# Products of constants in the waits of attention's tail and of the routing, and the sum of the MLP's lists moved into the first chunk

## The chip, the cores and the metric

The kernel runs on one core of one Trainium2 chip. A core has TensorE (matrix products into PSUM), VectorE, ScalarE and GpSimd, and queues that issue transfers (SyncE's above all). The engines run on their own and meet at semaphores. The metric is the device time of one launch in microseconds. Before the change it is 556.07 us, the median of three runs (555.29 to 556.83).

## The reference

Three layers, one behind the other, in float32:

```
attention: 2 batches, 8 heads, 768 positions, 64 wide; a position sees the first n_sink (4) keys
           and the last window (128); softmax; result as x[1536, 512]
experts:   tokens with x @ w_skip > 0 go to the expert e = argmax(x @ w_gate) of 8:
           x + p[e] * relu(x @ w1[e]) @ w2[e]        w1: 512 x 1024, w2: 1024 x 512
           the other tokens pass unchanged
MLP:       h = x @ w_in (512 x 2048); g = h if h > 0 else exp(h) - 1; out = g @ w_out
```

## The kernel before

**Attention** works on pairs of heads: 8 pairs times 6 tiles of 128 queries are 48 units (`UNITS`). TensorE's program for a unit u transposes its probabilities (`turn_unit`), makes the scores of unit u+2 (`qk`), at times transposes packed sinks (`turn_sinks`) and a finished block of x (`turn_x`), multiplies a block with the gate weights (`gate`), and does the products with the values of unit u-1 (`pv`). ScalarE and VectorE copy the transposed tiles from PSUM. Four more steps (`STEPS` = 52) drain this pipeline: in steps 46 and 47 no scores are left to make, in steps 50 and 51 only the last two gate products and the last transpose are left. Unit 0 and 1 already have fills (`early_fill`, L1403): products of a bf16 tile of ones with itself, 512 columns wide, into a PSUM tile that nobody reads.

**Routing** is a relay. VectorE finds each token's expert (`hot_b`); TensorE counts tokens per expert and ranks them (L1554 to L1562); VectorE turns ranks into slots, and for each of 12 token tiles makes a one-hot tile `here`; TensorE sums with it which token stands in each row of chunk 0 (L1571 to L1576), GpSimd gathers that chunk's rows into `xg`. VectorE then classifies tokens, TensorE ranks the classes (L1577 to L1585, for the order in which the MLP will read its rows), VectorE makes 12 more tiles `here`, and TensorE sums the other chunks' lists (L1587 to L1592). A chunk is 128 rows of one expert.

**Experts.** `turn(g)` transposes the gathered rows of chunk g, ScalarE copies them to `xg_t`. `chunk` (L1603) does 64 instructions of the up block (8 tiles of 128 hidden values, in float32), transposes the next chunk's rows, and does 24 products of the down block (each weight and each activation split into a high and a low part, three products each). In the first chunk the gates are summed between the up block and the transposes (`sum_gates`). Behind the first chunk, TensorE loads from memory how many chunks the first expert has, runs a loop over them if there is a second, and then sums the lists for the MLP: for 9 tiles, 18 products of `there` (a one-hot tile made by VectorE) into `ps_list`, which VectorE copies after chunk 0 (`keep_lists`, L1300). Then comes expert 1 (`expert(0, 1)`), which loads its first and last chunk and loops.

**The MLP** follows, in 4 blocks of 3 tiles.

The order on every engine is the order of its program text; nothing is scheduled at run time but the loops over chunks.

Of the kernel before, what the change touches and what calls it, by code (L numbers as in the profile page):

```python
# [22 lines left out]
def build(nc, q_t, k_s, v_p, n_sink, window, w_skip, w_gate, w1, w2, w_in, w_out, out):  # L23
# [86 lines left out]
    with ExitStack() as ctx:  # L110
# [1263 lines left out]
        def _(pe):  # L1374
# [41 lines left out]
            with pe.If(fits > 0):  # L1416

                def turn_unit(u):

                    pe.wait_ge(prob_ready, 2 * u + 2)  # L1420
                    if u >= 1:

                        pe.wait_ge(turned_a, u)
                        pe.wait_ge(turned_b, u)
                    if x_turned_at(u - 1) is not None:
                        pe.wait_ge(xt_kept, x_turned_at(u - 1) + 1)
                    if gate_at(u - 1) is not None:
                        pe.wait_ge(gate_added, gate_at(u - 1) + 1)
                    for h in range(2):
                        for m, (_, c) in enumerate(key_tiles(u % QT)):  # L1430
                            last = pe.transpose(ps_turn[h][:, m, :], prob_of(u, h)[:, c:c + P], identity[:])  # L1431
                    last.then_inc(unit_turned, 1)
# [50 lines left out]
                def sinks_pv(g):  # L1483

                    if g == 1:
# [3 lines left out]
                    pe.matmul(ps_pv[g % 2][:, 0:2 * PV], sink_t[:], v_sink[:, g // PG].rearrange("p i d -> p (i d)"),  # L1489
                              start=False, stop=True, skip_group_check=True).then_inc(group_done, 1)  # L1490

                for u in range(STEPS):
                    if u < 2:
                        early_fill(3 + u)
                    if u < UNITS:
                        turn_unit(u)
                    if u + 2 < UNITS:
                        qk(u + 2)
                    g = sinks_turned_at(u)
                    if g is not None:  # L1500
                        turn_sinks(u, g)
                    if gate_at(u) is not None:
                        gate(u, gate_at(u))
                    if x_turned_at(u) is not None:
                        turn_x(u, x_turned_at(u))
                    if 1 <= u <= UNITS:
                        pv(u - 1)
                    if g is not None:
                        sinks_pv(g)
            with pe.Else():  # L1510
# [27 lines left out]
                with pe.Fori(0, NT) as t:  # L1538
# [8 lines left out]
                                         start=(c == 0), stop=(c == DC - 1))  # L1547
                    last.then_inc(logits_ready, 1)

            pe.wait_ge(route_step, HOT)  # L1550
            pe.wait_ge(const_done, 9)
            rank = ps_rank[:, 0:NT * E].rearrange("p (t e) -> p t e", e=E)
            for t in range(NT):
                last = pe.matmul(ps_count[0:E, 0:NT], hot_b[:, t, :], ones[:, 0:NT], start=(t == 0), stop=(t == NT - 1))  # L1554
# [1 line left out]
            for t in range(NT - 1):  # L1556
                pe.matmul(rank[:, t + 1:, :], ones[:], hot_b[:, t:t + 1, :].broadcast_to([P, NT - 1 - t, E]),
                          start=(t == 0), stop=False, skip_group_check=True)
            pe.matmul(rank, tri[:], hot_b[:], start=False, stop=False, skip_group_check=True)
            pe.wait_ge(rows_ready, 1)  # L1560
            pe.matmul(ps_rank[:, 0:NT * E + E1], rows_b[0:E, :], below_b[0:E, :], start=False, stop=True,
                      skip_group_check=True).then_inc(ranks_ready, 1)  # L1562
# [2 lines left out]
            def turn(g):  # L1565
# [2 lines left out]
                    last = pe.transpose(ps_x[:, c, :], xg[:, c * P:(c + 1) * P], identity[:])  # L1568
                last.then_inc(xg_turned, 1)

            for t in range(NT):  # L1571
                pe.wait_ge(here_ready, t + 1)
                for m in range(2):
                    last = pe.matmul(ps_source[:, 0:1], here[:, t, :], token_id[:, m, t, :],
                                     start=(t == 0 and m == 0), stop=(t == NT - 1 and m == 1))
            last.then_inc(sources_summed, 1)  # L1576
            pe.wait_ge(order_step, CLASSED)  # L1577
            for t in range(ET - 1):
                pe.matmul(ps_place[:, t + 1:, :], ones[:], member[:, t:t + 1, :].broadcast_to([P, ET - 1 - t, E1]),
# [2 lines left out]
            for t in range(ET):  # L1582
                last = pe.matmul(ps_place, ones[:], lower[:, t:t + 1, :].broadcast_to([P, ET, E1]),
                                 start=False, stop=(t == ET - 1), skip_group_check=True)
            last.then_inc(places_ranked, 1)  # L1585
            pe.wait_ge(first_named, 1)
            for t in range(NT):  # L1587
                pe.wait_ge(here_ready, NT + t + 1)
                for m in range(2):
                    last = pe.matmul(ps_source[:, 0:CHUNKS], here[:, t, :], named[:, m, t, :],  # L1590
                                     start=(t == 0 and m == 0), stop=(t == NT - 1 and m == 1))
            last.then_inc(sources_summed, 1)  # L1592
            pe.wait_ge(routed, 1)
            pe.sem_inc(down_done, 1)
            turn(0)
            def sum_gates():
                pe.wait_ge(gates_named, 1)
                for t in range(NT):
                    last = pe.matmul(ps_gates[:, 0:3 * CHUNKS], here[:, t, :], gates_as[:, :, t, :],
                                     start=(t == 0), stop=(t == NT - 1))  # L1600
                last.then_inc(gates_summed, 1)

            def chunk(pair, half, g, first=False):  # L1603
                at = DOWN_AT[half]
# [7 lines left out]
                    last.then_inc(up_done, 1)  # L1612
                if first:
                    sum_gates()

                turn(g + 1)
                pe.wait_ge(y_copied, g + 1)
# [17 lines left out]
            with pe.If(second > 1):  # L1635
                with pe.Fori(1, second) as g:
                    chunk(0, 0, g)
            for t in range(ET):
                pe.wait_ge(there_ready, t + 1)
                for m in range(2):  # L1640
                    last = pe.matmul(ps_list, there[:, t, :], listed_as[:, m, t].rearrange("p k j -> p (k j)"),
                                     start=(t == 0 and m == 0), stop=(t == ET - 1 and m == 1))
            last.then_inc(lists_summed, 1)
            expert(0, 1)
            with pe.Fori(1, E // 2) as pair:
                for half in range(2):
# [134 lines left out]
```

## Time and profile before

| | |
|---|---|
| median of 3 runs | 556.07 us (555.29 to 556.83) |
| the profiled execution's own time | 555.49 us |
| its span (first to last instruction) | 553.7 us |
| mean granted clock of TensorE | 0.985 |
| TensorE busy, products / weight loads | 533.0 us (96%) / 462.4 us (84%) |
| VectorE / ScalarE / GpSimd busy | 271.1 / 216.3 / 50.7 us |
| chain that ended last | TensorE 89%, DMA 3%, VectorE 3%, issue 2%, ScalarE 2% |

Attention ends at about 138 us, the routing at about 154 us, the experts at about 277 us; the rest is the MLP. In the profile PE is TensorE's products, PEld its weight loads, DVE VectorE, ACT ScalarE, POOL GpSimd, SP SyncE. Times are in us from the start of the span; a wait in brackets behind an instruction is its engine's idle time before it, with what ended it. "issue" is time in which nothing that the profile shows was waited for. Ends of products are modelled, so that the length of one in a row of many is longer than its share of the row.

### The profile page before, as it was taken

The page shows a single profiled execution, that of the slowest core. Times are in us where ns is not written, and L with a number is a line of the kernel's source. Part 1 is how long each engine was busy: PE and PEld are TensorE (multiplying, and loading weights), DVE is VectorE, ACT ScalarE, POOL GpSimd, SP SyncE. Part 2 cuts the span into 40 slices and gives each one's busy share as a digit, 9 for nine tenths or more (in the row PEclk, how much of TensorE's full clock was granted, in tenths as well). Part 3 has the DMA queues.
Part 4 walks back from the last instruction along what each step waited for, and adds up shares of the span by engine and source line. Part 5 has one row for each costly group of instructions (what it writes and reads, how often), then busy time and mean ns, then how long its engine had stood idle before and what let it go on. Part 6 is the DMA issues. An engine that isn't in the chain of part 4 may idle for free.

```text
span 553.7 us, 8991 instructions
## 1 busy us (share of the span) xinstructions
PE 533.0 (96%) x3270; PEld 462.4 (84%) x3271; DVE 271.1 (49%) x726; ACT 216.3 (39%) x429; POOL 50.7 (9%) x108
## 2 busy tenths in 40 slices
PE   8999999998599999999999999999999999999997
PEld 4777777777388998998989899999999999999996
DVE  6566655553884345555766634333343333433332
ACT  4566565553043334445644423322233222332222
POOL 6000000000111101111220000400004000020000
PEclk9999999999589999999999999999999999999999
DMA  9468997322118559999952000200003000010001
GB/s 211 139 237 286 306 302 245 117 93 97 40 40 323 204 192 343 360 358 343 369 186 76 1 0 1 99 16 1 1 1 114 0 0 0 1 57 1 1 0 57
DMA packets 46956, 72.22 MB, mean 130 GB/s; under 512 B 16452, under 2 KB 16708, under 8 KB 46916
## 3 DMA queue, kind: packets, MB, share of 16 engines
q1 hardware_dynamic: 42018, 61.35, 32.6%
q0 software_dynamic: 2400, 7.87, 4.5%
q10 hardware_dynamic: 2498, 2.51, 1.3%
q8 instruction: 21, 0.34, 0.2%
q14 instruction: 19, 0.16, 0.1%
HBM read 57.56 MB, written 14.16 MB: 130 GB/s over the span
## 4 chain that ended last, share of the span: by engine, by line
PE 89%; DMA 3%; DVE 3%; issue 2%; ACT 2%; ACTq 0%; POOL 0%; POOLq 0%; DVEq 0%
PE ps_out L1690 24%; PE ps_g L1379 24%; PE ps_h L1610 9%; PE ps_y L1379 7%; PE ps_pv L1477 7%; PE ps_qk L1400 5%; PE ps_turn L1431 4%; DMA xg<-rows,source_i 3%; PE ps_turn L1459 2%; PE ps_pv L1489 1%; DVE prob L1045 1%; PE ps_turn L1447 1%; PE ps_x L1568 1%; PE ps_turn L1439 1%; PE ps_x L1653 1%
## 5 line engine op out<-in xcount | busy, mean ns | idle before, releaser
L1379 PE MATMUL ps_g<-x_hi,w_hi 128*128 128x384 f32 x252 | 85.1, 338 | 0.0
L1379 PE MATMUL ps_g<-x_lo,w_hi 128*128 128x384 f32 x252 | 84.8, 336 | 0.0
L1379 PE MATMUL ps_g<-x_hi,w_lo 128*128 128x384 f32 x252 | 84.7, 336 | 0.0
L956 ACT ACTIVATE g_raw<-ps_g 128x384 f32<-128x384 f32 x64 | 31.5, 492 | 125.7 <-PE ps_g L1379 123.0
L1353 DVE TENSOR_SCALAR g_raw<-g_raw 128x384 f32<-128x384 f32 x64 | 23.1, 361 | 117.3 <-ACT g_raw L956 117.3
L1690 PE MATMUL ps_out<-w_hi,g_hi 128*128 128x512 f32 x192 | 75.5, 393 | 0.2
L1690 PE MATMUL ps_out<-w_hi,g_lo 128*128 128x512 f32 x192 | 75.5, 393 | 0.0
L1690 PE MATMUL ps_out<-w_lo,g_hi 128*128 128x512 f32 x192 | 75.4, 393 | 0.0
L1610 PEld LDWEIGHTS ps_h<-xg_t,up_w 128*128 128x128 f32 x576 | 67.4, 196 | 2.8 <-issue 1.1
L1610 PE MATMUL ps_h<-xg_t,up_w 128*128 128x128 f32 x576 | 67.8, 280 | 1.7 <-issue 1.1
L960 ACT ACTIVATE g_hi<-g_raw 128x384 fp32r<-128x384 f32 x64 | 33.7, 526 | 62.2 <-DVE g_raw L1356 62.2
L1361 DVE TENSOR_TENSOR g_lo<-g_raw,g_hi 128x384 fp32r<-128x384 f32 x64 | 35.7, 558 | 36.1 <-ACT g_hi L960 36.1
L1379 PEld LDWEIGHTS ps_g<-x_hi,w_lo 128*128 128x128 f32 x252 | 47.4, 188 | 2.4
L1379 PEld LDWEIGHTS ps_g<-x_hi,w_hi 128*128 128x128 f32 x252 | 47.4, 188 | 2.3
L1477 PE MATMUL ps_pv<-v_pad,prob_t 128*128 128x130 f32 x352 | 49.0, 280 | 0.0
L824 ACT ACTIVATE prob<-prob,low 128x288 f32<-128x288 f32 (+1 forms) x96 | 43.6, 503 | 11.0 <-DVE low L1045 10.7
L1379 PEld LDWEIGHTS ps_g<-x_lo,w_hi 128*128 128x128 f32 x252 | 47.4, 188 | 0.0
L1477 PEld LDWEIGHTS ps_pv<-v_pad,prob_t 128*128 128x128 f32 x352 | 43.3, 192 | 3.8 <-ACT prob_t L838 3.1
L1045 DVE CUSTOM_DVE_ANT_0 prob<-ps_qk,bias 128x288 f32<-128x288 f32 (+1 forms) x96 | 38.5, 422 | 12.4 <-PE ps_qk L1400 11.5
L1690 PEld LDWEIGHTS ps_out<-w_hi,g_lo 128*128 128x128 f32 x192 | 36.1, 188 | 8.1
L1690 PEld LDWEIGHTS ps_out<-w_hi,g_hi 128*128 128x128 f32 x192 | 36.1, 188 | 6.4 <-ACT g_hi L960 0.5
L1690 PEld LDWEIGHTS ps_out<-w_lo,g_hi 128*128 128x128 f32 x192 | 36.1, 188 | 5.5
(192 smaller groups left out, 705.9 us busy)
## 6 DMA issues: line engine op xcount, KB each, us to landing
raw<-in_moe_w SPq DMA_DIRECT2D x16, 1024.0 KB, 6.6
up_w<-in_moe_w SPq DMA_DIRECT2D x16, 1024.0 KB, 10.4
raw<-in_moe_w_in SPq DMA_DIRECT2D x4, 1024.0 KB, 6.7
raw<-in_moe_w_out SPq DMA_DIRECT2D x4, 1024.0 KB, 7.2
rows<-zeros SPq DMA_DIRECT2D x2, 1792.0 KB, 9.4
v_pad<-in_v SPq DMA_DIRECT2D x16, 192.0 KB, 4.8
rows<-x_tok SPq DMA_DIRECT2D x6, 512.0 KB, 4.4
k_pair<-in_k SPq DMA_DIRECT2D x7, 432.0 KB, 4.1
```

The source lines that it names most:

```text
L824: act.activation(out_, out_, ACT.Exp, bias=low[:, n % 4:n % 4 + 1], scale=-1.0).then_inc(prob_ready, 1)
L956: act.activation(g_raw[f % GB][:], ps_g[f % 2][:, 0:TW], ACT.Exp).then_inc(g_exp_done, 1)
L960: act.activation(g_hi[f % GB][:], g_raw[f % GB][:], ACT.Copy).then_inc(g_hi_done, 1)
L1045: dve.tensor_tensor_reduce(out=prob_of(u, h), in0=ps_qk[n % 4][:, 0:w], in1=bias_of(u % QT), scale=-SCALE, scalar=BIG, op0=ALU.add, op1=AL ...
L1353: dve.tensor_scalar(g_raw[f % GB][:], g_raw[f % GB][:], 1.0, 1.0, ALU.min, ALU.subtract).then_inc(g_min_done, 1)
L1361: dve.tensor_tensor(g_lo[f % GB][:], g_raw[f % GB][:], g_hi[f % GB][:], ALU.subtract).then_inc(g_lo_done, 1)
L1379: last = pe.matmul(to, w, x, start=start and m == 0, stop=stop and m == 2)
L1400: pe.matmul(ps_qk[(2 * u + h) % 4][:, 0:w], q_pair[p % 2][rows, i * P:(i + 1) * P], k_pair[p % 2][rows, first:first + w], start=True, stop ...
L1431: last = pe.transpose(ps_turn[h][:, m, :], prob_of(u, h)[:, c:c + P], identity[:])
L1477: last = pe.matmul(ps_pv[g % 2][:, u % 2 * PV:(u % 2 + 1) * PV], prob_t[u % 2][:, h, m, :], v_pad[p % 2][h][:, tile, :], start=(u % 2 == 0 ...
L1610: last = pe.matmul(ps_h[i][:, f, :], up_w[half][i][:, c, f * P:(f + 1) * P], xg_t[:, c, :], start=(c == 0), stop=(c == DC - 1))
L1690: return pe.matmul(ps_out[i][:], act[f % GB][:, i * P:(i + 1) * P], weight, start=(f == 0 and act is g_hi and weight is high), stop=(f == ...
```

## The change

Five places on TensorE. `tail_fill` (3 products of ones, 512 columns, into `ps_qk[0]`) stands behind the transposes of steps 46, 47, 50 and 51. `fill(n)` (n products of ones by `tri`, 512 columns, into `ps_h[1]`) stands: 7 times ahead of the wait for `hot_b`, once ahead of the last rank product, 4 times ahead of each loop that sums `here` and ahead of the class ranks, once at every third tile of both loops, and twice ahead of the first transposes `turn(0)`. The wait for the constants (`const_done`) moves up. The 18 list products move from behind the first expert's loop into the first chunk, behind the gate sums (`sum_lists`).

```
--- before.py
+++ after.py
@@ -1489,11 +1489,18 @@
                     pe.matmul(ps_pv[g % 2][:, 0:2 * PV], sink_t[:], v_sink[:, g // PG].rearrange("p i d -> p (i d)"),
                               start=False, stop=True, skip_group_check=True).then_inc(group_done, 1)
 
+                def tail_fill():
+                    for _ in range(3):
+                        pe.matmul(ps_qk[0][:], ones[:], ones[:].rearrange("p (o k) -> p o k", o=1).broadcast_to([P, KP, P]),
+                                  start=True, stop=True)
+
                 for u in range(STEPS):
                     if u < 2:
                         early_fill(3 + u)
                     if u < UNITS:
                         turn_unit(u)
+                    if u in (UNITS - 2, UNITS - 1, UNITS + 2, UNITS + 3):
+                        tail_fill()
                     if u + 2 < UNITS:
                         qk(u + 2)
                     g = sinks_turned_at(u)
@@ -1547,8 +1554,14 @@
                                          start=(c == 0), stop=(c == DC - 1))
                     last.then_inc(logits_ready, 1)
 
+            def fill(n):
+                for _ in range(n):
+                    pe.matmul(ps_h[1][:], ones[:], tri[:].rearrange("p (o k) -> p o k", o=1).broadcast_to([P, KP, P]),
+                              start=True, stop=True)
+
+            pe.wait_ge(const_done, 9)
+            fill(7)
             pe.wait_ge(route_step, HOT)
-            pe.wait_ge(const_done, 9)
             rank = ps_rank[:, 0:NT * E].rearrange("p (t e) -> p t e", e=E)
             for t in range(NT):
                 last = pe.matmul(ps_count[0:E, 0:NT], hot_b[:, t, :], ones[:, 0:NT], start=(t == 0), stop=(t == NT - 1))
@@ -1557,6 +1570,7 @@
                 pe.matmul(rank[:, t + 1:, :], ones[:], hot_b[:, t:t + 1, :].broadcast_to([P, NT - 1 - t, E]),
                           start=(t == 0), stop=False, skip_group_check=True)
             pe.matmul(rank, tri[:], hot_b[:], start=False, stop=False, skip_group_check=True)
+            fill(1)
             pe.wait_ge(rows_ready, 1)
             pe.matmul(ps_rank[:, 0:NT * E + E1], rows_b[0:E, :], below_b[0:E, :], start=False, stop=True,
                       skip_group_check=True).then_inc(ranks_ready, 1)
@@ -1568,12 +1582,16 @@
                     last = pe.transpose(ps_x[:, c, :], xg[:, c * P:(c + 1) * P], identity[:])
                 last.then_inc(xg_turned, 1)
 
+            fill(4)
             for t in range(NT):
+                if t % 3 == 2:
+                    fill(1)
                 pe.wait_ge(here_ready, t + 1)
                 for m in range(2):
                     last = pe.matmul(ps_source[:, 0:1], here[:, t, :], token_id[:, m, t, :],
                                      start=(t == 0 and m == 0), stop=(t == NT - 1 and m == 1))
             last.then_inc(sources_summed, 1)
+            fill(4)
             pe.wait_ge(order_step, CLASSED)
             for t in range(ET - 1):
                 pe.matmul(ps_place[:, t + 1:, :], ones[:], member[:, t:t + 1, :].broadcast_to([P, ET - 1 - t, E1]),
@@ -1583,8 +1601,11 @@
                 last = pe.matmul(ps_place, ones[:], lower[:, t:t + 1, :].broadcast_to([P, ET, E1]),
                                  start=False, stop=(t == ET - 1), skip_group_check=True)
             last.then_inc(places_ranked, 1)
+            fill(4)
             pe.wait_ge(first_named, 1)
             for t in range(NT):
+                if t % 3 == 2:
+                    fill(1)
                 pe.wait_ge(here_ready, NT + t + 1)
                 for m in range(2):
                     last = pe.matmul(ps_source[:, 0:CHUNKS], here[:, t, :], named[:, m, t, :],
@@ -1592,6 +1613,7 @@
             last.then_inc(sources_summed, 1)
             pe.wait_ge(routed, 1)
             pe.sem_inc(down_done, 1)
+            fill(2)
             turn(0)
             def sum_gates():
                 pe.wait_ge(gates_named, 1)
@@ -1599,6 +1621,14 @@
                     last = pe.matmul(ps_gates[:, 0:3 * CHUNKS], here[:, t, :], gates_as[:, :, t, :],
                                      start=(t == 0), stop=(t == NT - 1))
                 last.then_inc(gates_summed, 1)
+
+            def sum_lists():
+                for t in range(ET):
+                    pe.wait_ge(there_ready, t + 1)
+                    for m in range(2):
+                        last = pe.matmul(ps_list, there[:, t, :], listed_as[:, m, t].rearrange("p k j -> p (k j)"),
+                                         start=(t == 0 and m == 0), stop=(t == ET - 1 and m == 1))
+                last.then_inc(lists_summed, 1)
 
             def chunk(pair, half, g, first=False):
                 at = DOWN_AT[half]
@@ -1612,6 +1642,7 @@
                     last.then_inc(up_done, 1)
                 if first:
                     sum_gates()
+                    sum_lists()
 
                 turn(g + 1)
                 pe.wait_ge(y_copied, g + 1)
@@ -1635,12 +1666,6 @@
             with pe.If(second > 1):
                 with pe.Fori(1, second) as g:
                     chunk(0, 0, g)
-            for t in range(ET):
-                pe.wait_ge(there_ready, t + 1)
-                for m in range(2):
-                    last = pe.matmul(ps_list, there[:, t, :], listed_as[:, m, t].rearrange("p k j -> p (k j)"),
-                                     start=(t == 0 and m == 0), stop=(t == ET - 1 and m == 1))
-            last.then_inc(lists_summed, 1)
             expert(0, 1)
             with pe.Fori(1, E // 2) as pair:
                 for half in range(2):
```

## Rows read from the trace of the kernel before

**Rows 1.** Page, the span in 40 slices: granted clock of TensorE in tenths.

```profile
PEclk9999999999589999999999999999999999999999
```

**Rows 2.** Windows of 1 us: busy us (count) per engine, then granted clock, DMA share, GB/s.

```profile
139.00:140.00 1.00, 0.00 (x0) 0.00 (x0) 0.51 (x2) 0.00 (x0) 0.00 (x0) 1.00 0.12 43
...
140.00:141.00 1.00, 0.00 (x0) 0.00 (x0) 0.86 (x4) 0.28 (x1) 0.00 (x0) 0.81 0.02 8
...
151.00:152.00 1.00, 1.00 (x13) 0.67 (x11) 1.00 (x6) 0.00 (x0) 0.00 (x0) 0.50 0.00 0
...
157.00:158.00 1.00, 1.00 (x8) 1.00 (x7) 0.93 (x5) 0.00 (x0) 0.00 (x0) 0.65 0.57 98
```

**Rows 3.** Timeline of TensorE, 126 to 154: start, length, line, operands, count, idle before.

```profile
129.59 0.30 PE L1439 MATMUL ps_turn<-identity,sink_p 128*128 128x128 f32 x1 [0.52 <-issue]
...
132.28 0.58 PE L1459 MATMUL ps_turn<-wg,xt_sb 128*128 128x9 f32 x4 [0.56 <-issue]
...
136.62 0.61 PE L1459 MATMUL ps_turn<-wg,xt_sb 128*128 128x9 f32 x4 [0.47 <-ACT xt_sb L846]
...
137.97 0.61 PE L1459 MATMUL ps_turn<-wg,xt_sb 128*128 128x9 f32 x4 [0.47 <-ACT xt_sb L846]
...
141.22 0.45 PE L1554 MATMUL ps_count<-ones,hot_b 128*8 128x12 bf16 x12 [2.63 <-DVE hot_b L1204]
...
142.38 0.27 PE L1561 MATMUL ps_rank<-below_b,rows_b 8*128 8x105 bf16 x1
...
143.81 2.37 PE L1574 MATMUL ps_source<-token_id,here 128*128 128x1 bf16 x24 [1.17 <-DVE here L1228]
...
147.41 0.48 PE L1579 MATMUL ps_x<-member,ones 128*128 128x72 bf16 x8 [1.23 <-DVE lower L1239]
...
149.93 2.29 PE L1590 MATMUL ps_source<-named,here 128*128 128x20 bf16 x24 [1.34 <-DVE here L1254]
```

**Rows 4.** Chain of waits, 125 to 180 us: start, length, what held the chain.

```profile
152.22 0.98 PE ps_x L1568 x4
...
153.87 9.22 PE ps_h L1610 x64
...
163.09 0.33 PE ps_gates L1599 x12
...
163.42 0.47 PE ps_x L1568 x4
...
169.49 0.46 PE ps_x L1641 x18
...
169.95 1.06 issue
...
171.00 7.38 PE ps_h L1610 x64
```

**Rows 5.** Timeline of TensorE in the later experts.

```profile
197.41 7.31 PE L1610 MATMUL ps_h<-xg_t,up_w 128*128 128x128 f32 x64
...
218.14 0.66 PE L1568 MATMUL ps_x<-identity,xg 128*128 128x128 f32 x4 [0.23 <-DMA xg<-rows,source_i]
```

**Rows 6.** Timeline of TensorE, 0 to 12 us: the fills.

```profile
1.00 3.41 PE L1405 MATMUL ps_pv<-ones 128*128 128x512 bf16 x8 [1.00 <-POOL ones L688]
...
5.56 0.82 PE L1405 MATMUL ps_pv<-ones 128*128 128x512 bf16 x3
...
7.78 1.04 PE L1405 MATMUL ps_pv<-ones 128*128 128x512 bf16 x4
```

**Rows 7.** Timeline of VectorE, 142 to 160 us.

```profile
142.08 0.24 DVE L1217 TENSOR_SCALAR rows_b<-chunk_rows,n_chunks 8x128 bf16<-8x128 bf16 x1
...
143.47 2.44 DVE L1228 TENSOR_SCALAR here<-lane,slot 128x128 bf16<-128x128 f32 x12
...
154.53 0.24 DVE L1274 TENSOR_TENSOR placed<-ps_x,member 128x81 f32<-128x81 f32 x1 [0.39 <-issue]
...
157.47 1.85 DVE L1290 TENSOR_SCALAR there<-lane,lane_in 128x128 bf16<-128x128 f32 x9
```

More of the change, by code:

```diff
@@ L1490, in sinks_pv, with tail_fill @@
                               start=False, stop=True, skip_group_check=True).then_inc(group_done, 1)
+                def tail_fill():
+                    for _ in range(3):
+                        pe.matmul(ps_qk[0][:], ones[:], ones[:].rearrange("p (o k) -> p o k", o=1).broadcast_to([P, KP, P]),
+                                  start=True, stop=True)
                 for u in range(STEPS):
@@ L1496, in _ @@
                         turn_unit(u)
+                    if u in (UNITS - 2, UNITS - 1, UNITS + 2, UNITS + 3):
+                        tail_fill()
                     if u + 2 < UNITS:
@@ L1548, in _, with fill @@
                     last.then_inc(logits_ready, 1)
+            def fill(n):
+                for _ in range(n):
+                    pe.matmul(ps_h[1][:], ones[:], tri[:].rearrange("p (o k) -> p o k", o=1).broadcast_to([P, KP, P]),
+                              start=True, stop=True)
+            pe.wait_ge(const_done, 9)
+            fill(7)
             pe.wait_ge(route_step, HOT)
-            pe.wait_ge(const_done, 9)
             rank = ps_rank[:, 0:NT * E].rearrange("p (t e) -> p t e", e=E)
@@ L1559, in _ @@
             pe.matmul(rank, tri[:], hot_b[:], start=False, stop=False, skip_group_check=True)
+            fill(1)
             pe.wait_ge(rows_ready, 1)
@@ L1569, in turn @@
                 last.then_inc(xg_turned, 1)
+            fill(4)
             for t in range(NT):
+                if t % 3 == 2:
+                    fill(1)
                 pe.wait_ge(here_ready, t + 1)
@@ L1576, in _ @@
             last.then_inc(sources_summed, 1)
+            fill(4)
             pe.wait_ge(order_step, CLASSED)
@@ L1585, in _ @@
             last.then_inc(places_ranked, 1)
+            fill(4)
             pe.wait_ge(first_named, 1)
             for t in range(NT):
+                if t % 3 == 2:
+                    fill(1)
                 pe.wait_ge(here_ready, NT + t + 1)
@@ L1594, in _ @@
             pe.sem_inc(down_done, 1)
+            fill(2)
             turn(0)
@@ L1601, in sum_gates, with sum_lists @@
                 last.then_inc(gates_summed, 1)
+            def sum_lists():
+                for t in range(ET):
+                    pe.wait_ge(there_ready, t + 1)
+                    for m in range(2):
+                        last = pe.matmul(ps_list, there[:, t, :], listed_as[:, m, t].rearrange("p k j -> p (k j)"),
+                                         start=(t == 0 and m == 0), stop=(t == ET - 1 and m == 1))
+                last.then_inc(lists_summed, 1)
             def chunk(pair, half, g, first=False):
@@ L1614, in chunk @@
                     sum_gates()
+                    sum_lists()
                 turn(g + 1)
@@ L1637, in _ @@
                     chunk(0, 0, g)
[L1638 to L1643, printed above, removed]
             expert(0, 1)
```

## The prediction

> **What bounds the kernel now.** I read the page first: TensorE is busy nearly throughout, and its granted clock is at nine tenths or more in every slice but two, which read 5 and 8 [rows 1]. Then windows of 1 us around those two slices: TensorE does nothing between 139 and 140 us, the mean clock of the next window is 0.81, that of 151 to 152 is 0.50, and that of 157 to 158 is 0.65 [rows 2]. With only two levels, 1.2 and 2.4 GHz, the fall is at about 140.6 us (0.62 of that window at full speed) and the rise at about 157.7 us. Before the fall the engine had its last gate product at 137.97 to 138.58 and then a wait of 2.63 us [rows 3]; the rise came after almost 4 us of the unbroken first up block.
>
> Then the chain of waits through this stretch. The first up block (64 instructions) takes 9.22 us, the second, the same work at full clock, 7.38 [rows 4]: 1.84 us go to the clock. After the list products stands a gap of 1.06 us named issue, before the second block. The tail of attention and the routing are a relay between engines: TensorE's waits there are 0.52, 0.56, 0.47, 0.47, 2.63, 1.17, 1.23 and 1.34 us [rows 3], each ended by VectorE, ScalarE or issue. From 171 us on TensorE is the bound, with one recorded wait for a gathered block of 0.23 us near 218 us [rows 5], so what is won before 171 us should reach the end.
>
> **The price of a fill.** The same product (ones by ones, 128x512, bf16) stands at the start of the kernel. Three take 0.82 us and four 1.04, so one more costs 0.22; eight in a row take 3.41, so about 0.42 each [rows 6]. I read those as the price at full and at low clock (the clock column there shows 1.00; it is the duration that says otherwise).
>
> **1. Fills in attention's tail: 4 times 3.** They go behind the transposes of units 46 and 47 and ahead of the last two gate products. Each group is 3 x 0.22 = 0.66 us at full clock, and the instruction behind it starts at the later of its releaser and the fill's end. Waits of 0.52, 0.56, 0.47 and 0.47 leave 0.14 + 0.10 + 0.19 + 0.19 = 0.62 us uncovered. The cover is ScalarE's and VectorE's copies out of PSUM, which don't depend on the fills; all that queues behind is TensorE's own, and the routing waits for its last gate product. Bounds: 0 (the releases slip less than I think, as the modelled ends make possible) to 2.64 (nothing covered). I take +0.62, since the four wait rows are these very places.
>
> **2. Fills in the routing.** fill(7) is 1.54 us in a wait of 2.63: nothing at full clock, up to +0.31 at 0.42 each. fill(1) ahead of the rank product: the rows of chunks that this product needs come from VectorE at 142.08 + 0.24 = 142.32 [rows 7], while the product starts at 142.38. TensorE's eleven rank products before it run cold in this trace, and warm they leave about the room of one fill: 0, at worst +0.22. fill(4) is 0.88 us, in waits of 1.17, 1.23 and 1.34: 0 each. In the two loops that sum lists, VectorE makes 12 tiles in 2.44 us [rows 7], one every 0.20 us. Three tiles give 0.59 us; the six products of three tiles at full clock cost about what the gates' twelve show, 0.33 / 12 = 0.03 each [rows 4], so 0.17, and with a fill 0.39. VectorE stays the pace, except at the last tile: the pair before it and its fill, 0.06 + 0.22, end 0.08 after the tile is made. fill(2) before the first transposes is on the path (0.44), because the gathered rows wait for TensorE there and not the reverse: +0.44.
>
> **3. What full clock gives back in the routing.** The four transposes and their release take 0.98 us cold against 0.47 when warm (the same four at 163.42) [rows 4]: -0.51. The count products, the rank product behind them and the lag of the first list sum behind VectorE are each a few tenths long and mostly latency; I give them -0.15 together, bounds 0 and -0.4. With fill(2) and the 0.08, parts 2 and 3 come to 0.44 + 0.08 - 0.51 - 0.15 = -0.14.
>
> **4. The first up block.** -1.84 us, if the clock never falls. Bounds: 0 (it is low as before) and -7.4 (in another execution the whole block might be cold, 2 x 7.38 against 7.38). The median of the runs shown (556.07) is 0.58 above the profiled execution's 555.49, and they spread by 1.5; part of that may be a longer cold stretch, which a held clock would remove too.
>
> **5. The list products into the first chunk.** 18 products, 0.46 us [rows 4], stand now behind the gate sums instead of behind the first down block: the same time on TensorE, 0. They wait for nothing: VectorE ends their nine selectors at 157.47 + 1.85 = 159.32 [rows 7], with the shift of part 1 about 159.8, and TensorE gets there at about 153.87 + 0.62 - 0.14 + 7.38 + 0.33 = 162.0. If that cover of 2.2 us were gone, queued behind the wait would be the transposes of the next block, then ScalarE's copy, and the down block. What the move may save is the 1.06 us of issue. At later changes of expert (the one at 197.41 for all of them) the same two loads of bounds and the loop head stand right behind 24 long products and no gap is recorded [rows 5]; here they stand behind short ones. Once the lists are gone, the loads for the second chunk's test, the test, the two loads and the loop head all lie behind long products. On VectorE two such loads show as 0.39 us [rows 7], so the whole is some 1 to 2.5 us of TensorE's sequencer against a cover that I can't read. The gap after is between 0 and about 1.5; I take 0.4, nearest to the later experts' rows, so -0.66.
>
> The Trainium skill, TensorE: Matmul & The Clock Gate (section "Architectural detail", engine queue depths), gives this engine a queue of 64. By that, the sequencer would already be some 5 us ahead behind the down block and the lists with it; loads of 0.2 us each could not make the gap, something else would, and the move would not remove it: -0 in place of -0.66, a sum of -1.4. No row here shows the depth.
>
> **Sum.** +0.62 - 0.14 - 1.84 + 0 - 0.66 = -2.02 us. From the profiled execution: span 553.7 to 551.7, time 555.49 to 553.5. The median of the runs shown would give 554.05; since I put most of the 0.58 between the two down to a longer cold stretch, which goes as well, I stay close to the first: **553.6 us**, -0.45%. Its own range is 552.5 to 554.9.
>
> **Rivals.**
> (a) The clock is held, but the gap stays and the tail's fills are dearer (0.2 more each, because each sits between a release and its wait): +1.4 - 0.14 - 1.84 + 0 = -0.6, 554.9 from the profiled execution. For it: a TensorE chain that has no slack in the tail, and a gap whose cause no row names. Against: the waits measured at these places.
> (b) The clock still falls late: fills cover only a half to two thirds of each wait, with 1-column products between them, and what activity suffices no row shows. If it falls after most fills are through, and the up block starts low: +0.62 + 0.3 + 0 - 0.66 = +0.3, 555.8 from the profiled execution and 556.4 from the median, say 556.1. For it: from 144 to 152 us the engine is recorded as busy for most of the time in this trace and stays at half clock. Against: the product of ones fills the array with 512 columns, and the start of the kernel is held at the high level with 3 and 4 of them.
> (c) Slower: the clock falls early, as before, at the start of the routing. From there a fill costs 0.42. fill(1) puts the rank product back 0.38. fill(4) is 1.7 against 1.17. In the first loop TensorE alone has 2.37 + 4 x 0.42 = 4.05 us of work against VectorE's 2.44 and becomes the pace. Up to the first sum that is +2.2 us, up to the first transposes +5.7; the dense cold fills would then bring the clock back earlier, worth up to -1.84 and part of those 5.7. Net between +0.5 and +3.7, about 558. It decides as soon as cold fills on the path (0.42 each; some 20 lie there) eat the 2.7 us of gains, so from 7 or more. For it: the fall needed only 2 us of rest in this trace. Against: fill(7) starts at the very place where that rest began.
> (d) The gains meet a transfer: in the experts the weights fill the DMA engines, and gathered rows once came 0.23 us late [rows 5]. Everything that triggers those transfers moves along, so at most some tenths to 1 us are given back: 554.4.
>
> **How the numbers follow.** Forecast 0.55, (a) 0.13, (b) 0.09, (c) 0.17, (d) 0.06. A difference of 0.3% (1.67 us, so below 554.4 or above 557.7) is about what can be told from none. Of the forecast 0.48 lies below 554.4, of (a) and (d) 0.04; of (c) 0.13 lies above 557.7, and 0.02 of (a) and (b). Faster 0.52, same 0.33, slower 0.15. The range to leave no more than 0.2 out: 552.3 (some cold stretches of other executions saved as well) to 557.3, which takes in (a), (b), (d) and the lower part of (c).
>
> **What would show it.** In the trace of the changed kernel: windows of 1 us from 138 to 160 with clock 1.00 throughout; the first up block at 7.4 us; the fills 0.22 apart; the last gate product about 0.6 us later than now (137.97); VectorE's two loops of twelve still 2.44 us and no wait of VectorE for the sums above 0.3; the list products directly behind the gate sums; the gap before the second up block under 1 us. A clock of 0.50 in any of those windows would make the forecast wrong by (b) or (c), an unchanged gap by (a), and waits for gathered rows or weights after 171 us by (d).

## The result, and the profile after

The changed kernel takes 552.42 us, the median of 4 runs (551.88 to 552.90), against 555.68 for the kernel before in the 4 runs beside them (555.21 to 556.83); the ratio of the compared runs is 0.9925, 95% interval 0.9907 to 0.9942, so -0.75% (the two medians alone differ by 3.26 us, 0.59%). The forecast was 553.6 us, -0.45%, with a range of 552.3 to 557.3. Applied to the 556.07 us that the forecast started from, the ratio gives 551.9, below that range. The change helped, and by the two mechanisms forecast (a clock that holds, a gap that goes), but the gain was larger: one term of the sum, a price for the tail's fills, wasn't there at all, and the gap was worth more than I gave it.

The page's clock row of the changed kernel, to set against [rows 1]: the two low slices are gone, and the mean granted clock of the run is 1.0 against 0.985. In windows of 1 us from 136 to 182 us it is 1.00 in each.

```profile
PEclk9999999999999999999999999999999999999999
```

TensorE's timeline of the changed kernel through the same stretch, to set against [rows 3] (start, length, line, operands, count, idle before it). This execution is some 1.25 us late from its first ten microseconds on, so compare distances and not times.

```profile
129.71 0.60 PE L1431 MATMUL ps_turn<-identity,prob 128*128 128x128 f32 x4
...
130.14 0.81 PE L1494 MATMUL ps_qk<-ones 128*128 128x512 bf16 x3
...
130.83 0.30 PE L1439 MATMUL ps_turn<-identity,sink_p 128*128 128x128 f32 x1
...
139.23 0.60 PE L1459 MATMUL ps_turn<-wg,xt_sb 128*128 128x9 f32 x4
...
139.68 1.67 PE L1559 MATMUL ps_h<-tri,ones 128*128 128x512 bf16 x7
...
142.46 0.45 PE L1567 MATMUL ps_count<-ones,hot_b 128*8 128x12 bf16 x12 [1.10 <-DVE hot_b L1204]
...
145.00 0.40 PE L1591 MATMUL ps_source<-token_id,here 128*128 128x1 bf16 x4 [0.20 <-DVE here L1228]
...
148.66 0.38 PE L1597 MATMUL ps_x<-member,ones 128*128 128x72 bf16 x8 [0.34 <-DVE lower L1239]
...
151.17 0.32 PE L1611 MATMUL ps_source<-named,here 128*128 128x20 bf16 x4 [0.84 <-DVE here L1254]
...
153.37 0.59 PE L1559 MATMUL ps_h<-tri,ones 128*128 128x512 bf16 x2
...
155.09 7.41 PE L1640 MATMUL ps_h<-xg_t,up_w 128*128 128x128 f32 x64 [0.69 <-ACT xg_t L899]
...
162.66 0.60 PE L1629 MATMUL ps_x<-listed_as,there 128*128 128x18 bf16 x18
...
169.19 7.31 PE L1640 MATMUL ps_h<-xg_t,up_w 128*128 128x128 f32 x64
```

The reader is to see this. From the last gate product to the count products are 3.23 us (142.46 - 139.23) against 3.25 before: seven fills lie in the wait and cost nothing. From the last gate product to the first up block are 15.86 against 15.90, so what the other fills of the routing cost and what the full clock gives back there cancel; e9 below takes the two apart. The first up block takes 7.41 us against 9.22 [rows 4]. And the second up block (169.19) has no idle time in front of it, where it had 1.06 us; the list products stand behind the gate sums. Start to start, the kernel before has 1.67 us from the list products to the second up block (171.00 - 169.33):

```profile
169.33 0.61 PE L1641 MATMUL ps_x<-listed_as,there 128*128 128x18 bf16 x18
```

The list products themselves take 0.46 of these at either place, so the move saves 1.21 us: the printed 1.06, and 0.15 at the end of the last list product, which the printed gap leaves out.

From the last gate product to the second up block that is 29.96 us against 33.03 before, -3.07; from there to the MLP's first product 107.28 against 108.16, -0.88; from there to the end 274.6 against 274.5. The MLP's first product, before and after:

```profile
279.16 0.41 PE L1665 MATMUL ps_g<-x_hi,w_hi 128*128 128x384 f32 x1 [0.83 <-ACT x_hi L937]
...
276.47 0.41 PE L1690 MATMUL ps_g<-x_hi,w_hi 128*128 128x384 f32 x1 [0.83 <-ACT x_hi L937]
```

The spans differ by less (551.1 against 553.7, -2.6) because the profiled execution of the changed kernel lost 1.26 us more before the last gate product, nearly all of it in the first 10 us, which the change doesn't touch. Its start, with [rows 6] for the kernel before:

```profile
1.00 3.60 PE L1405 MATMUL ps_pv<-ones 128*128 128x512 bf16 x8 [1.00 <-POOL ones L688]
...
5.04 1.37 PE L1400 MATMUL ps_qk<-k_pair,q_pair 64*128 64x128 f32 x8
...
6.34 0.82 PE L1405 MATMUL ps_pv<-ones 128*128 128x512 bf16 x3
```

The eight products and the first scores run longer here (5.04 to 6.34 us for the scores, 4.65 to 5.56 before). I read that as a longer stretch at low clock: a fill there takes about 0.42 us, as fills at low clock do further on (e10), though the clock column shows 1.00 at the start of every trace.

### The profile page after: what moved, and what is told of

It is laid out like the page before. It is cut to its first block, busy times and chain, and to the rows that moved or that the text cites. A ratio compares the mean times of both kernels' runs of the same rounds, so it can differ in the third digit from the quotient of the medians.

```text
span 551.1 us, 9074 instructions
## 1 busy us (share of the span) xinstructions
PE 537.2 (97%) x3312; PEld 463.2 (84%) x3313; DVE 271.8 (49%) x726; ACT 216.2 (39%) x429; POOL 50.5 (9%) x108
## 4 chain that ended last, share of the span: by engine, by line
PE 94%; DVE 3%; issue 1%; ACT 1%; ACTq 0%; POOL 0%; DVEq 0%; POOLq 0%
PE ps_out L1715 24%; PE ps_g L1379 24%; PE ps_h L1640 12%; PE ps_y L1379 9%; PE ps_pv L1477 7%; PE ps_qk L1400 6%; PE ps_turn L1431 4%; PE ps_turn L1459 2%; PE ps_pv L1489 1%; DVE prob L1045 1%; PE ps_turn L1447 1%; PE ps_x L1582 1%; PE ps_x L1678 1%; PE ps_turn L1439 1%; PE ps_pv L1405 1%
## 5 line engine op out<-in xcount | busy, mean ns | idle before, releaser
L1640 PEld LDWEIGHTS ps_h<-xg_t,up_w 128*128 128x128 f32 x576 | 65.6, 192 | 1.6 <-ACT xg_t L899 0.9
L1640 PE MATMUL ps_h<-xg_t,up_w 128*128 128x128 f32 x576 | 65.9, 275 | 0.7 <-ACT xg_t L899 0.7
```

The source lines that it names most:

```text
L1640: last = pe.matmul(ps_h[i][:, f, :], up_w[half][i][:, c, f * P:(f + 1) * P], xg_t[:, c, :], start=(c == 0), stop=(c == DC - 1))
```

## The experiments

All times are medians in us; "before" is the kernel before in the runs beside it on the same chip; G is the distance in the trace from the last gate product to the second up block, U the length of the first up block, X the distance from the second up block to the MLP's first product. Cold and warm stand for TensorE at its lower granted clock (1.2 GHz, 0.50 in the rows) and at full clock (2.4 GHz, 1.00).

| kernel | time | before | ratio (95%) | G | U | X |
|---|---|---|---|---|---|---|
| before, first trace | | 555.68 | | 33.03 | 9.22 | 108.16 |
| before again (e5) | 556.86 | 556.72 | 1.000 (0.9989 to 1.0012) | 33.30 | 9.49 | 108.58 |
| before, third (e14) | 557.03 | 556.56 | 1.001 (0.9998 to 1.0023) | 33.61 | 9.85 | 107.60 |
| changed, first trace | 552.42 | 555.68 | 0.9925 (0.9907 to 0.9942) | 29.96 | 7.41 | 107.28 |
| changed again (e6) | 553.02 | 556.72 | 0.9933 (0.9919 to 0.9946) | 29.99 | 7.41 | 107.54 |
| changed, third (e16) | 552.42 | 556.56 | 0.9930 (0.9913 to 0.9947) | 29.97 | 7.41 | 107.27 |
| lists only (e1) | 554.49 | 557.18 | 0.9952 (0.9936 to 0.9969) | 32.37 | 9.77 | 108.01 |
| lists only again (e15) | 554.96 | 556.56 | 0.9978 (0.9965 to 0.9991) | 31.75 | 9.14 | 107.75 |
| fills only (e2) | 553.61 | 557.18 | 0.9945 (0.9929 to 0.9960) | 31.14 | 7.41 | 107.31 |
| changed, no tail fills (e3) | 552.97 | 557.18 | 0.9930 (0.9916 to 0.9945) | 29.98 | 7.41 | 107.75 |
| changed, tail fills only (e4) | 554.87 | 557.18 | 0.9957 (0.9942 to 0.9973) | 32.41 | 9.73 | 107.27 |
| tail fills of six (e7) | 555.12 | 556.72 | 0.9975 (0.9961 to 0.9989) | 29.90 | 7.41 | 107.34 |
| lists ahead of the test (e8) | 556.86 | 556.72 | 0.9993 (0.9981 to 1.0006) | 32.30 | 7.41 | 108.95 |
| no fill on the path (e9) | 551.90 | 556.68 | 0.9931 (0.9905 to 0.9956) | 29.47 | 7.41 | 107.27 |
| no tail fills, no seven (e10) | 553.73 | 556.68 | 0.9953 (0.9938 to 0.9967) | 31.01 | 7.41 | 107.26 |
| no loop fills (e11) | 555.37 | 556.68 | 0.9964 (0.9943 to 0.9985) | 32.42 | 9.11 | 107.27 |
| only the seven (e12) | 554.57 | 556.68 | 0.9967 (0.9953 to 0.9981) | 31.99 | 9.43 | 107.96 |
| fills in waits alone (e13) | 552.50 | 556.56 | 0.9922 (0.9905 to 0.9938) | 29.49 | 7.41 | 107.49 |

**The two parts one at a time.** e1 is the kernel before with only the lists moved, e15 the same once more; e2 has only the fills.

```
 e1, e15: chunk():  sum_gates()                e2: chunk():  sum_gates()
+                   sum_lists()                    (behind the first expert's loop:)
         no fills                                  sum_lists()
                                               +   all fills
```

> The kernel before with the list products moved into the first chunk, no fills. Theory L (TensorE's sequencer runs only a short lead ahead, and the 1.06 us of issue is its loads of bounds standing behind short products): the gap before the second up block goes, and nothing takes its place, -1.1 us (-0.2%); the clock still falls near 140 us and the first up block stays at 8.5 to 11 us. Rival Q (the sequencer is far ahead, the gap has another cause): the gap stays near 1.06 and the time is that of the kernel before.

> All the fills, the list products at their old place. If the parts add: clock 1.00 throughout, first up block 7.4 us, gap of 1.0 to 1.1 us before the second up block; -1.8 to -2.5 us (-0.4%). If the fills gave nothing by themselves: the time of the kernel before.

In e1 the gap is gone and in e2 it stays:

```profile
165.56 0.60 PE L1607 MATMUL ps_x<-listed_as,there 128*128 128x18 bf16 x18
...
172.11 7.31 PE L1618 MATMUL ps_h<-xg_t,up_w 128*128 128x128 f32 x64
```

```profile
167.84 0.61 PE L1629 MATMUL ps_x<-listed_as,there 128*128 128x18 bf16 x18
...
169.46 7.38 PE L1640 MATMUL ps_h<-xg_t,up_w 128*128 128x128 f32 x64 [1.00 <-issue]
```

The clock of e1 is low from 143.5 to 160.6 us, its first up block 9.77 us long; the trace of e2 is at full clock throughout. By distance G, e2 is 1.18 us above the changed kernel: the gap of 1.00 and the end of the last list product. What theory L expects came out, what Q expects did not. The -2.7 us timed for e1 is more than its trace explains; that is taken up below.

**What makes the gap.** In e8 the lists stand between the first chunk and the load and test for a second chunk.

```
             chunk(0, 0, 0, first=True)
+            sum_lists()
             second = pe.value_load(base_i[0:1, 1:2], ...)
```

> All the fills; the list products stand right behind the first chunk, ahead of the load and the test for a second chunk (in the kernel before they stand between the test and expert 1). Theory L (short lead): the load, the test, the two loads and the loop head all stand behind short products, so the gap before the second up block grows from 1.0 to 1.5 to 2.5 us; +1.5 to +2.5 us over the changed kernel. Rival Q (the gap has another cause): it stays at 1.0.

```profile
168.78 0.61 PE L1629 MATMUL ps_x<-listed_as,there 128*128 128x18 bf16 x18
...
171.54 9.01 PE L1640 MATMUL ps_h<-xg_t,up_w 128*128 128x128 f32 x64 [2.15 <-issue]
```

Windows of 1 us in the same trace:

```profile
172.00:173.00 1.00, 1.00 (x9) 1.00 (x8) 0.00 (x0) 0.00 (x0) 0.00 (x0) 0.71 1.15 365
...
175.00:176.00 1.00, 1.00 (x7) 1.00 (x7) 0.00 (x0) 0.00 (x0) 0.00 (x0) 0.58 1.03 389
```

The gap is 2.15 us: the load and test add 1.15 to the 1.00 of two loads and a loop head. Behind the 24 long products of the down block the whole of it is hidden (e1, and the changed kernel). So where the loads stand decides the gap. That TensorE's sequencer (which works through loads, branches and loop heads) is only a short way ahead of the products when short ones come before it is the reading that fits; no row shows the sequencer itself. The clock fell once more: these two windows put the fall at 172.4 us, just behind this rest, and the rise at 175.8. That made the second up block 9.01 us long (X is 108.95); in time e8 gives back everything and equals the kernel before.

**Which fills hold the clock.** e3 leaves out the tail's, e4 has these alone, e12 has only the seven, e11 lacks those in the two loops.

```
 e3:  -  if u in (UNITS - 2, UNITS - 1, UNITS + 2, UNITS + 3): tail_fill()
 e4:  -  fill(7), fill(1), fill(4) x3, fill(1) at every third tile, fill(2)
 e12: as e4, but  + fill(7)  and  - tail_fill()
 e11: -  if t % 3 == 2: fill(1)        (both loops)
```

> The changed kernel without the four groups of three fills in attention's tail; those of the routing stay. Theory T (the tail's fills are needed, since the last microseconds before the long wait are thin): the clock falls near 140 us or soon after, fills at 0.42 us lie on the path, and the time is 1 to 4 us above the changed kernel. Rival R (the seven fills in the long wait and those behind are enough): clock 1.00, time equal to the changed kernel within 0.1%; its tail no shorter, if the fills lay wholly in waits there.

> The changed kernel with the tail's fills alone; none in the routing. I expect the clock to fall all the same, at 140 to 145 us, the first up block at 8.5 to 11 us, so +1.8 to +3 us over the changed kernel, about the time of the lists-only kernel. If the tail alone held the clock through the routing: the time of the changed kernel.

> The changed kernel with no fills but the seven in the long wait of 2.6 us, and with the lists moved. If that wait alone costs the clock: 1.00 throughout, up block 7.4, -0.5 us against the changed kernel. If the whole routing is too thin (I lean to this): the clock falls one to several microseconds later than in the kernel with the lists moved and no fills, and the up block is above 8.5 us, the time within 0.5 us of that kernel.

> The changed kernel without the single fills in the two loops over 12 tiles; the groups of 7, 4, 4, 4, 2 and the one ahead of the rank product stay. If the loops' own small products keep the clock: 1.00, and -0.1 us. If they don't (I lean to this: 2.4 us with products 1 or 20 columns wide): the clock falls inside or just behind one of the loops and the up block is above 8 us; +1 to +3 us.

Windows of 1 us (busy per engine, granted clock, DMA share, GB/s), the one in which the clock falls: e4, e12, e11.

```profile
143.00:144.00 1.00, 0.94 (x24) 0.90 (x24) 0.55 (x4) 0.00 (x0) 0.00 (x0) 0.77 0.00 0
```

```profile
144.00:145.00 1.00, 1.00 (x11) 0.61 (x12) 1.00 (x6) 0.00 (x0) 0.00 (x0) 0.82 0.00 0
```

```profile
149.00:150.00 1.00, 1.00 (x13) 0.59 (x10) 0.93 (x3) 0.00 (x0) 1.00 (x1) 0.60 0.00 0
```

e3 keeps 1.00 in every window and a mean clock of 1.0 in all five executions, and its tail is no shorter: rival R, as far as five executions show. e4 falls at about 143.5 us and e12 at about 144.6 us against their last gate products at 139.74 and 138.20; e11 gets through the first loop and the class ranks, falls at about 149.2 us, and its first up block takes 9.11 us. So neither the tail's fills nor the seven are enough, and with all groups in place those between small products in the loops are still needed; the later groups were not taken out one by one. e11's executions differ: mean granted clock 0.997 in four (551.6 to 552.9 us) and 0.990 to 0.994 in eight (555.3 to 556.5). Even 0.997 is not a clock that held: e8 has that mean with 3.4 us at low clock. So in e11 the clock fell in all twelve, and chance decides for how long and at what cost.

Whether the tail can do without fills in every execution stays open, though. In the third trace of the kernel before (e14) the clock fell at 139.8 us, while the last gate product was still running and before the long wait had begun:

```profile
139.23 0.61 PE L1459 MATMUL ps_turn<-wg,xt_sb 128*128 128x9 f32 x4 [0.47 <-ACT xt_sb L846]
```

```profile
139.00:140.00 1.00, 0.61 (x4) 0.52 (x4) 0.12 (x1) 0.17 (x1) 0.00 (x0) 0.89 1.00 377
...
140.00:141.00 1.00, 0.00 (x0) 0.00 (x0) 0.32 (x3) 0.00 (x0) 0.00 (x0) 0.50 0.38 141
```

Of the seven fills hardly one would have started by then (in the first trace of the changed kernel they start 0.45 us behind that product's start). That execution has a mean clock of 0.982, against 0.984 or 0.985 in the eleven others of e14. Of all executions of the kernel before and of lists only that the record lists with a clock, 7 of 125 are as low (0.981 or 0.982), so the case is rare, and the five executions of e3 may simply not have met it.

**The forecast's rival (c), made on purpose.** e10 has neither the tail's fills nor the seven, but all the later ones.

> The changed kernel without the tail's fills and without the seven in the long wait; the later ones (1, 4, loops, 4, 4, loop, 2) stay. This is the forecast's rival (c) made on purpose: the clock falls in the long wait, and what follows runs into fills at 0.42 us each. By that rival the first up block then starts 3 to 6 us later against the last gate product than in the changed kernel, and the time is that of the kernel before or worse. Rival H: the dense fills bring the clock back within a few microseconds, the up block is warm at 7.4 us, and the loss stays under 2 us against the changed kernel.

```profile
140.00:141.00 1.00, 0.00 (x0) 0.00 (x0) 0.90 (x4) 0.24 (x1) 0.00 (x0) 0.67 0.02 8
...
147.00:148.00 1.00, 1.00 (x7) 0.28 (x5) 0.78 (x4) 0.00 (x0) 0.38 (x2) 0.92 0.00 0
```

```profile
141.23 0.44 PE L1564 MATMUL ps_count<-ones,hot_b 128*8 128x12 bf16 x12 [2.72 <-DVE hot_b L1204]
...
142.91 1.89 PE L1557 MATMUL ps_h<-tri,ones 128*128 128x512 bf16 x4
...
144.59 0.29 PE L1588 MATMUL ps_source<-token_id,here 128*128 128x1 bf16 x4
...
154.78 7.41 PE L1637 MATMUL ps_h<-xg_t,up_w 128*128 128x128 f32 x64 [0.69 <-ACT xg_t L899]
```

The clock falls at about 140.3 us, as in the first trace of the kernel before, and is back at about 147.2, not at 157.7: rival H. The low-clock fills (four in 1.68 us, 0.42 each) put the first up block back by 1.02 us against the changed kernel (16.88 against 15.86 behind the last gate product), and the block itself is warm, 7.41. That is 1 us, not the 3 to 6 of rival (c).

**What the tail's fills cost.** e7 has six in each group instead of three.

```
 def tail_fill():
-    for _ in range(3):
+    for _ in range(6):
```

> The changed kernel with six products instead of three in each of the four groups of the tail. Theory D (the idle time that the timeline prints begins at the modelled end of the instruction before, some 0.16 us after the array is free, so that a wait printed as 0.47 to 0.56 holds three fills of 0.22): three were free and each of the next three costs its 0.22, so the last gate product stands 4 x 0.66 = 2.6 us later against the start of unit 46, and the time is +2.6 us (+0.5%). Rival: the fills in the tail are free for another reason (the tail has slack elsewhere), and six cost well under 2 us.

TensorE's timeline of e7 at unit 46 and at the last gate product:

```profile
128.43 0.60 PE L1431 MATMUL ps_turn<-identity,prob 128*128 128x128 f32 x4
...
128.87 1.46 PE L1494 MATMUL ps_qk<-ones 128*128 128x512 bf16 x6
...
130.16 0.27 PE L1439 MATMUL ps_turn<-identity,sink_p 128*128 128x128 f32 x1
...
140.17 0.51 PE L1459 MATMUL ps_turn<-wg,xt_sb 128*128 128x9 f32 x4
```

From the transposes of unit 46 to the last gate product are 11.74 us against 9.52 in the changed kernel, +2.22, so of 2.64 us added 0.42 were still covered. With three they cost nothing: the same distance in the kernel before is 9.50, its transposes standing at

```profile
128.47 0.60 PE L1431 MATMUL ps_turn<-identity,prob 128*128 128x128 f32 x4
...
129.59 0.30 PE L1439 MATMUL ps_turn<-identity,sink_p 128*128 128x128 f32 x1 [0.52 <-issue]
```

and the sink's transpose 1.12 us behind, the same 1.12 as in the changed kernel (129.71 to 130.83). The four transposes fill the array for 0.44 us (the first fill starts 0.43 behind them), so 0.68 us are free, where the timeline prints 0.52: it counts from the modelled end of the fourth, an estimated 0.16 us late. Theory D stands. Two of e7's twelve executions have a mean clock of 0.993 and take 556.8 us; where it fell in them no trace shows.

**Only fills that a wait covers.** e9 drops the two ahead of the first transposes and the one ahead of each loop's last tile; e13 does so too and puts 11, 5 and 7 where 7, 4 and 4 stood.

```
 e9:  -  fill(2)                                    e13: as e9, and
      -  if t % 3 == 2: fill(1)                      -  fill(7)   fill(4)   fill(4)
      +  if t % 3 == 2 and t < NT - 1: fill(1)       +  fill(11)  fill(5)   fill(7)
```

> The changed kernel without the two products ahead of the first transposes and without the one ahead of the last tile in each of the two loops that sum lists; these are the fills that no wait covers. Theory P (the clock doesn't need them): clock 1.00, first up block starts 0.45 to 0.65 us earlier against the last gate product, -0.5 us (-0.1%). Rival: the clock falls somewhere behind 150 us and the up block takes over 8 us.

> The changed kernel with no fill that a wait doesn't cover (none ahead of the first transposes, none ahead of a loop's last tile), and more where the changed kernel's trace still shows idle time: 11 for 7 in the long wait, 5 for 4 ahead of the class ranks, 7 for 4 ahead of the second loop. From the last gate product to the second up block 29.4 to 29.5 us as in the kernel without the fills on the path, no run with a cold stretch, and -0.5 us against the changed kernel, -4.2 against the one before. If the added fills are not covered: up to +0.2 per fill.

Both traces have the first up block 15.36 or 15.37 us behind the last gate product, 0.5 less than the changed kernel, at clock 1.00. But one of e9's six runs had a mean clock of 0.993 and took 555.74 us, against 551.06 to 552.97 for the others. All 16 executions of the changed kernel have 1.0, which would fit that the dropped fills cover such a case; but e7 has these fills and shows 0.993 in two of twelve, so that isn't shown. None of e13's six runs is below 1.0, which is too few to tell. In time e13 (0.9922) can't be told from the changed kernel beside it (0.9930), since the intervals overlap; the 0.5 us is shown by the traces alone.

**Repeats: what of the gain is chance.**

> The kernel before, unchanged, for a second trace of it. In the five traces so far the first scores start at 4.65 to 5.04 us and the last gate product at 137.97 to 139.74 us, with the first products at 0.42 us each for shorter or longer. Theory S (the start costs 0 to 1.8 us by the moment at which the clock rises, and the first up block 9.2 to 9.8, in any kernel): ratio 1.00, last gate product anywhere from 138 to 139.8, up block above 9. Rival: the trace repeats to 0.1 us, and the spread of the times comes from elsewhere.

> The changed kernel, unchanged, beside the kernel before on one chip. From the last gate product to the second up block 29.96 us again (33.03 before); ratio 0.993 to 0.994. The start may differ by up to 1.8 us (theory S).

> The kernel before, unchanged, a third trace. Theory G (the waits for gathered rows belong to the kernel before, from its gap or its cold block): second up block to the MLP's first product 108.0 to 108.6 us again, with a wait recorded. Rival: 107.3 as often as 108, so chance.

> The lists-only kernel, unchanged. If its gain of 2.7 us was in part chance: now 1.1 to 2 us (ratio 0.9965 to 0.998). If it stays near 0.995, more than the gap comes with the lists; then the trace should show it behind the second up block (107.3 us to the MLP's first product against 108.0).

> The changed kernel, unchanged, a third trace: 29.9 to 30.0 us from the last gate product to the second up block, 107.3 to 107.5 from there to the MLP's first product, ratio 0.993 to 0.994.

The last gate product stands at 137.97, 139.31 and 139.23 us in the three traces of the kernel before, and at 139.23, 139.70 and 137.99 in those of the changed one: theory S, the start costs up to 1.7 us by chance. The cold up block takes 9.22, 9.49 and 9.85; the warm one 7.41 every time. Lists only gains 1.2 us on repeat (0.9978), as its gap says. The intervals of e1 and e15 only just meet (0.9965 to 0.9969), and e1's trace shows nothing more than the gap, so I take the rest of its 2.7 us as chance. X is 107.60 to 108.58 in the kernel before and 107.27 to 107.54 in the changed one. e5's trace shows where such time goes, to a wait for gathered rows:

```profile
220.54 0.66 PE L1568 MATMUL ps_x<-identity,xg 128*128 128x128 f32 x4 [1.03 <-DMA xg<-rows,source_i]
```

But e14 has no such wait recorded, and with a cold routing e4 has 107.27 while with a warm one e3 has 107.75, so theory G is not shown: the means of three traces each differ by 0.75 us, and the cause stays open.

## Why the prediction was too small

What failed is the price of the tail's fills (step 1) and the size of the gap (step 4): +0.62 and -0.66 in the sum, +0.02 and -1.21 in the traces. The rest of the shortfall is a cold block that is usually longer than in the one trace I had (step 3) and a part whose cause stays open (step 5). By its steps, the kernel before to the changed one, traces for traces.

1. **Tail fills, +0.62: failed.** Measured +0.02 (9.50 to 9.52 us over the stretch). I subtracted the printed idle times from 0.66; these begin at a modelled end some 0.16 us after the array is free (worked out above from start-to-start distances), so that three fills find 0.68 us and not 0.52. In the five executions of e3 the clock didn't need them either; e14 leaves open whether a rarer execution does.
2. **Fills and warm products in the routing, -0.14: right to a tenth** (-0.04). The cost of fill(2), 0.43 in the trace, is paid back by warmer transposes (their start to the up block's is 1.78 before and 1.29 after, -0.49) as worked out; the -0.15 that I gave the small products isn't there, since the second list loop starts 11.96 us behind the last gate product before and 11.94 after. e9 shows the 0.5 us that the uncovered fills cost.
3. **First up block, -1.84: right for the profiled execution** (-1.81), too small for the usual one. Against the three traces before it is -1.81, -2.08 and -2.44. I had seen that the median of runs lay above the profiled execution, and gave it too little.
4. **Lists, 0 and gap -0.66: mis-sized.** The whole gap went, 1.06 us as printed and 1.21 start to start. I bounded the sequencer's work at 1 to 2.5 us and its cover as unknown; in e8 2.15 of it show, and 24 long products (5.6 us) cover it. The sentence that I based on the Trainium skill (TensorE: Matmul & The Clock Gate, "Architectural detail", a queue of 64), that the gap would then stay, was a wrong inference: the gap went in e1 and grew in e8, with nothing but the place of the list products changed. No run here measures the depth.
5. **Everything behind moves rigidly: nearly.** A further -0.3 to -1.0 us of X (trace for trace: -0.88, -1.04, -0.33), cause open.

The forecast of the sum was -2.02 us on the profiled execution. The same terms measured are 0.02 - 0.04 - 1.81 - 1.06 = -2.89; with the end of the last list product (0.15) and rounding, G falls by 3.07; by the means of three traces each G falls by 3.3 (33.31 to 29.97) and X by 0.75, together -4.1. The three timed ratios say -3.7 to -4.2 (the medians of the first alone -3.3). Of the rivals, (a) fell with the changed kernel's own trace and e1, and (b) is what e11 shows when the loops are left bare. The mechanism of (c) exists, but at 1 us and not 3 to 6 (e10), because the clock came back early. For (d) the reverse was seen: a wait for gathered rows is recorded in two of three traces of the kernel before and in none of the changed one.

## What to carry to other kernels

Where the granted clock falls, try cheap full-width products in the waits along the whole thin stretch. Here the long wait alone was not enough, and the small products of the loops didn't replace them. Size them by start-to-start distances rather than by the idle time that a timeline prints. Put loads of loop bounds and branches on TensorE behind long products: behind 18 short ones they stood bare here, for 1.0 to 2.15 us. And look at the granted clock of every execution, not only of the profiled one: a rare fall shows only there.

## What was not expected

- Fills at the low clock can be a remedy and not only a cost: with some ten of them between the small products the clock came back after 6.8 us (140.3 to 147.2, e10), without them after 17.1 (140.6 to 157.7, the kernel before), though TensorE was recorded as busy for most of that stretch there. Six were not enough in e11 (four at 149.3 us, two at 153.3): its clock was back at 159.4. In all seven traces with no fill behind the fall the rise came 3.7 to 5.1 us into the first up block.
- The clock fell again 0.9 us behind a rest of 2.15 us between a run of short list products and the second up block (e8), while the same kernel's wait of 1.10 us ahead of the count products, behind seven fills, left it at 1.00. In e14 it fell with no rest above 0.56 us in the 10 us before.
- The start of the kernel, the same in all of them, varies from execution to execution (the last gate product stands at 137.97 to 139.70 us in six traces), by the length of its stretch of slow products; two profiled executions can differ by 1.7 us before the change is reached.
